# Gate logits with one load of the high half: 24 products a block in place of 36, and one more VectorE instruction

## The chip, the cores and the metric

The kernel runs on one core of one Trainium2 chip. The metric is the device time of one execution in microseconds. Five engines run side by side, each with a queue of its own: TensorE (PE in the rows, with its weight loads as PEld), VectorE (DVE), ScalarE (ACT), GpSimd (POOL) and SyncE (SP, which here only issues DMAs). They meet through semaphores alone.

## The reference, cut to what matters

Three layers follow each other: a linear attention over 4 x 8 heads, an MLP over 2304 rows (512 to 2048 to 512), and a mixture of 8 experts of which each row uses one. The change is in the gate of the third layer, which reads the MLP's result `x` (2304 x 512):

```
logits = x @ w_gate                                  # 512 x 8
e_idx  = argmax(logits, axis=1)
probs  = softmax(logits)                             # with + 1e-09 in the divisor
gate_w = probs[row, e_idx]
eom    = 1 / (1 + exp(-(x @ w_output_gate)))         # 512 x 8
out[row] = gate_w * eom[row, e_idx] * (relu(x[row] @ w1[e]) @ w2[e])     # e = e_idx[row]
```

Both small matrices lie side by side in the kernel, so that a row has 2 x 8 = 16 gate columns.

## The kernel before, in words

**Numbers as two halves.** float32 operands of the large products are split into two float16 halves, a high one and what is left of it, the low one. A product of two such operands is three products: high by high, high by low, low by high (`PARTS = ((0, 0), (0, 1), (1, 0))`, L328). For the gate, `yt` holds the transposed rows in both halves, `wg_sb` the 16 gate columns in both.

**The MLP's blocks.** The 2304 rows go in `BLOCKS` = 6 blocks of 384 rows (`BT` = 3 row tiles of 128). In `mlp_block` each block has 16 steps f, one for each 128 columns of the hidden layer. On TensorE a step is `hidden` two steps ahead (12 products of 384 columns, L898) and `output` (9 products of 512 columns, L909). Between them ScalarE makes a relu (L1249), VectorE the gated product (`gate_chunk`, L1650), ScalarE its high half (L1260), and VectorE its low half (`gate_lo`, L1655), for which `output` waits. TensorE needs VectorE's result two `hidden` calls later.

**What VectorE has beside it.** In the same steps VectorE prepares the experts' weights, three units of 128 x 4096 words a block: `unit_search` (L1569), `unit_scale` (L1584 to L1587) and `unit_lo` (L1594). ScalarE makes the units' high halves (L1237) and its queue waits for `unit_scale` before the first of them. At the end of a block VectorE finds the rows' largest values (`row_scales`, L1534 to L1542), and early in the next it makes the rows' low halves (L1561).

**The gate.** A block's gate is worked out within the next block: `y_logits(n - 1)` on TensorE after the `output` of step 8 (L925 to L940), `route_first` on VectorE in step 10 (L1607 to L1623), `ranks` on TensorE after the `output` of step 10 (L942), `route_second` on VectorE in step 12 (L1625 to L1645). In the last block of the MLP these come two steps sooner. The gate of the last block itself stands between the first two expert tiles. The order within each engine's queue is written out by hand. Blocks 1 to 4 are a loop of two blocks a turn, with 0 and 5 outside it.

Every instruction of the two route functions adds one to the semaphore `route` and the next waits for it; `ROUTE` is the count of a block, `ONEHOT` and `ARGS` are the counts at which `ranks` and ScalarE's two exponentials may start (L72, L943, L1226). All gate results lie in PSUM bank 7 (`LB`): 48 columns of logits from column 0, the ranks from column 128.

**After the MLP** come up to 27 tiles of 128 rows, each through its expert: `slot_hidden` (L994, 96 products of 128 columns) and `slot_output` (L1006, 24 products of 512 columns).

The functions in which the change lies:

Of the kernel before, what the change touches and what calls it, by code (L numbers as in the profile page):

```python
# [22 lines left out]
ALU = mybir.AluOpType  # L23
RMAX = bass.bass_isa.ReduceOp.max
ACT = mybir.ActivationFunctionType
AX = mybir.AxisListType

P = 128
# [3 lines left out]
E, EF = 8, 1024  # L32
# [10 lines left out]
BT = 3  # L43
BLOCKS = TILES // BT
BN = BT * P
DC = DM // P
# [22 lines left out]
SOON = (0, 1, 2, FC - 1)  # L69
W_UP = 3  # L70
YSTEPS, YUP = 6, 4
ONEHOT, ARGS, ROUTE = 6, 8, 21  # L72
NOWHERE = 2 * N


def moe_program(nc, qkt_in, v, w_phi, w_in, w_out, w_gate, w_ogate, w1, w2, out, rows, split, recs):
    ctx = ExitStack()

    def sb(name, shape, dt=F32):
        return ctx.enter_context(nc.sbuf_tensor(name, shape, dt))  # L80
# [4 lines left out]
    with ctx:  # L85

        ps = ctx.enter_context(nc.psum_tensor("ps", [P, 8, 512], F32))
# [3 lines left out]
        wg_sb = sb("wg_sb", [P, 2, DC, 2 * E], F16)  # L91
# [75 lines left out]
        yt = y_words[:, 0:DC * BN].bitcast(F16).rearrange("p (l c n) -> p l c n", l=2, c=DC)  # L167
# [26 lines left out]
        y_log = sb("y_log", [P, BT])  # L194
# [3 lines left out]
        lg = sb("lg", [P, BT, 2 * E])  # L198
# [129 lines left out]
        PARTS = ((0, 0), (0, 1), (1, 0))  # L328
# [8 lines left out]
        YB, HB, XB, LB = 0, (3, 4, 5), 6, 7  # L337
# [385 lines left out]
        def _(pe):  # L723
# [201 lines left out]
            def y_logits(n):  # L925

                if isinstance(n, int) and n == BLOCKS - 1:
                    pe.wait_ge(yt_ready, DC)
                else:
                    pe.wait_ge(yt_turned, n * (16 * BT) + 16 * BT)  # L930
                if not isinstance(n, int) or n == 0:
                    pe.wait_ge(low_copied, PAIRS)
                    pe.wait_ge(high_copied, PAIRS)
                pe.wait_ge(route, n * ROUTE + 1)
                for r in range(BT):
                    for c in range(DC):
                        for ly, lw in PARTS:
                            last = nc.tensor.matmul(ps[:, LB, r * 2 * E:(r + 1) * 2 * E], yt[:, ly, c, r * P:(r + 1) * P], wg_sb[:, lw, c, :],
                                                    start=c == 0 and ly + lw == 0, stop=c == DC - 1 and ly == 1)
                last.then_inc(logits_done, 1)  # L940

            def ranks(n):  # L942
# [5 lines left out]
            def mlp_block(n, a, post, more=True, ahead=0):  # L948
                first = isinstance(n, int) and n == 0
                pe.wait_ge(xs_hi, n + 1)  # L950
                pe.wait_ge(xs_lo, n + 1)
                if first:
                    pe.wait_ge(consts_made, 2)
                    pe.wait_ge(piece_hi, PAIRS // 2 - 1)
                    pe.wait_ge(piece_lo, PAIRS // 2 - 1)
                    pe.wait_ge(piece_hi_out, PAIRS // 2 - 2)
                    pe.wait_ge(piece_lo_out, PAIRS // 2 - 2)
                hidden(n, a, 0)
                hidden(n, a, 1)
                for f in range(FC):  # L960
                    if first and f + 2 == FC // 2:
                        pe.wait_ge(piece_hi, PAIRS // 2)
                        pe.wait_ge(piece_lo, PAIRS // 2)
                        pe.wait_ge(piece_hi_out, PAIRS // 2)
                        pe.wait_ge(piece_lo_out, PAIRS // 2)
                    if f + 2 < FC:
                        hidden(n, a, f + 2)
                    if not more and f == FC - 1:
                        pe.wait_ge(pos_ready, BLOCKS - 1)
                        for s in range(2):  # L970
                            slot_transposes(s, s, 1, (XB, LB)[s])
                    output(n, f)
                    if post and f == Y_AT + 5 - ahead:
                        y_logits(n - 1)
                    if post and f == Y_AT + 7 - ahead:
                        ranks(n - 1)
# [40 lines left out]
            n = BLOCKS - 1  # L1017
# [11 lines left out]
            pe.wait_ge(yt_ready, 1)  # L1029
            slot_output(0, 0, 0, (0,))  # L1030
            y_logits(n)
            slot_output(0, 0, 0, (1,))
            ranks(n)
# [269 lines left out]
        def _(dve):  # L1303
# [293 lines left out]
            def linker(start):  # L1597

                at = [start]

                def link(n, ins):
                    at[0] += 1
                    ins.then_inc(route, 1)
                    dve.wait_ge(route, n * ROUTE + (1 + at[0]))
                return link, at

            def route_first(n):  # L1607

                link, at = linker(0)
                dve.wait_ge(logits_done, n + 1)  # L1610
                link(n, nc.vector.tensor_tensor(lg[:], ps[:, LB, 0:BT * 2 * E].rearrange("p (r e) -> p r e", r=BT),
                                                y_log[:, :, None].to_broadcast([P, BT, 2 * E]), ALU.mult))
                link(n, nc.vector.tensor_reduce(r_mx[:], lg[:, :, 0:E], AX.X, ALU.max))
                link(n, nc.vector.tensor_tensor(r_a[:], lg[:, :, 0:E], r_mx[:, :, None].to_broadcast([P, BT, E]), ALU.subtract))

                link(n, nc.vector.scalar_tensor_tensor(out=r_b[:], in0=r_a[:], scalar=0.0, in1=iota8[:], op0=ALU.is_ge, op1=ALU.mult))
                link(n, nc.vector.tensor_reduce(r_s[:, 1, :], r_b[:], AX.X, ALU.min))
                link(n, nc.vector.tensor_tensor(onehot[:], iota8[:], r_s[:, 1, :, None].to_broadcast([P, BT, E]), ALU.is_equal))
                assert at[0] == ONEHOT
                link(n, nc.vector.tensor_tensor(r_b[:], onehot[:], lg[:, :, E:2 * E], ALU.mult))  # L1620
                link(n, nc.vector.tensor_reduce(r_s[:, 0, :], r_b[:], AX.X, ALU.add))
                assert at[0] == ARGS
                link(n, nc.vector.tensor_copy(yrow_words[:, :, DM + 1].bitcast(I32), token[:, bass.ds(n * BT, BT)]))  # L1623
# [70 lines left out]
            def mlp_block(n, a, post, units=3, ahead=0):  # L1694
                for f in range(FC):
# [37 lines left out]
                    if post and f == Y_AT + 7 - ahead:  # L1733
                        route_first(n - 1)
# [45 lines left out]
            slot_lo(0, 0, (3, 2))  # L1780
            slot_in(2, 0)
            route_first(BLOCKS - 1)
            route_second(BLOCKS - 1)
            slot_out(0, 0, None)
# [5 lines left out]
            def link(ins):  # L1790
                made[0] += 1
                ins.then_inc(table_step, 1)
                dve.wait_ge(table_step, made[0])
# [103 lines left out]
```

## Time and profile before

| | |
|---|---|
| median of 3 runs | 830.22 us (828.48 to 830.37) |
| the profiled execution | 827.24 us |
| its span, first to last instruction | 825.6 us |
| granted TensorE clock, mean | 0.996 |
| TensorE busy | 802.2 us (97%) |
| VectorE busy | 560.5 us (68%) |
| ScalarE busy | 393.0 us (48%) |

The span is cut into the attention (up to about 185 us), the MLP's blocks (185 to 567 us) and the experts' tiles. A busy share is a mean over all three. In 40 slices of about 20.6 us each, VectorE is at eight or nine tenths through the MLP's part, and below four tenths in most slices after it.

### The profile page before, as it was taken

What the parts mean: (1) busy time and instruction counts of PE and PEld (TensorE: products, weight loads), DVE (VectorE), ACT (ScalarE), POOL (GpSimd) and SP (SyncE); (2) the same over time, 40 slices, a digit from 0 to 9 for tenths busy, and PEclk for the clock granted to TensorE, in tenths of its full rate; (3) what the DMA queues carried; (4) which work ended last, traced back from release to release, by engine and by line L of the source; (5) the groups of instructions that cost most, each with busy time, mean ns of one, the idle gap of its engine ahead of it and who ended that gap; (6) DMA issues with size and microseconds to landing.
All of it is one profiled execution on the core that took longest, in us unless ns stands there. A gap on an engine that the chain in (4) does not pass through costs nothing.

```text
span 825.6 us, 19432 instructions
## 1 busy us (share of the span) xinstructions
PE 802.2 (97%) x7126; PEld 496.9 (60%) x7127; DVE 560.5 (68%) x1140; ACT 393.0 (48%) x857; POOL 179.9 (22%) x204
## 2 busy tenths in 40 slices
PE   7999999999999999999999999999999999999995
PEld 5666656655555555555555555556767777777773
DVE  5788798897978988888898897845723453222221
ACT  5888898883644644645646546434101121001110
POOL 4556666660000001010000001010211322111100
PEclk9999999999999999999999999999999999999998
DMA  7466677746656656855764756383273926266600
GB/s 237 148 204 206 213 237 207 215 143 219 233 204 217 228 206 220 262 210 207 217 253 167 246 219 208 135 343 142 83 278 142 378 65 237 78 231 248 235 28 14
DMA packets 67449, 164.37 MB, mean 199 GB/s; under 512 B 28614, under 2 KB 32966, under 8 KB 60736
## 3 DMA queue, kind: packets, MB, share of 16 engines
q1 hardware_dynamic: 61472, 146.74, 52.4%
q0 software_dynamic: 5760, 16.80, 5.7%
q8 instruction: 36, 0.59, 0.3%
q14 instruction: 21, 0.17, 0.1%
q10 hardware_dynamic: 160, 0.07, 0.0%
HBM read 114.16 MB, written 47.55 MB: 196 GB/s over the span
## 4 chain that ended last, share of the span: by engine, by line
PE 67%; DVE 16%; issue 10%; ACT 4%; DMA 1%; POOL 1%; SPq 1%; DVEq 0%; ACTq 0%; POOLq 0%
PE ps L909 17%; PE ps L898 15%; PE ps L994 11%; PE ps L1006 11%; PE ps L747 3%; DVE u_mx L1569 3%; DVE arena L1594 2%; PE ps L777 2%; PE ps L810 2%; DVE y_words L1561 1%; DVE arena L1320 1%; DVE arena L1337 1%; DVE relu L1650 1%; PE ps L984 1%; ACT arena L1112 1%
## 5 line engine op out<-in xcount | busy, mean ns | idle before, releaser
L898 PE MATMUL ps<-arena,w_in_sb 128*128 128x384 f16 x1152 | 200.9, 326 | 0.0
L909 PE MATMUL ps<-w_out_sb,arena 128*128 128x512 f16 x576 | 171.3, 379 | 1.5 <-DVE stage L1655 1.5
L898 PEld LDWEIGHTS ps<-arena,w_in_sb 128*128 128x128 f16 x1152 | 111.8, 98 | 81.1 <-issue 0.2
L1288 ACT ACTIVATE x_t<-ps 128x512 f16<-128x512 f32 x54 | 31.6, 596 | 200.3 <-PE ps L994 175.0
L994 PE MATMUL ps<-x_t,arena 128*128 128x128 f16 x2112 | 121.5, 219 | 2.0 <-issue 1.9
L994 PEld LDWEIGHTS ps<-x_t,arena 128*128 128x128 f16 x2112 | 119.2, 98 | 5.9 <-issue 2.6
L1006 PE MATMUL ps<-arena,x_t 128*128 128x512 f16 x528 | 117.9, 379 | 0.0
L909 PE MATMUL ps<-w_out_sb,stage 128*128 128x512 f16 x288 | 109.1, 379 | 0.0
L1260 ACT ACTIVATE arena<-relu 128x384 f16<-128x384 f32 x96 | 50.0, 521 | 119.1 <-DVE relu L1650 119.1
L909 PEld LDWEIGHTS ps<-w_out_sb,arena 128*128 128x128 f16 x576 | 55.7, 98 | 61.9 <-issue 4.8
L1762 DVE SCALAR_TENSOR_TENSOR x_t<-ps,x_t 128x512 f16<-128x512 f32 x54 | 36.7, 690 | 78.9 <-ACT x_t L1288 78.9
L1112 ACT ACTIVATE arena<-ps,arena 128x128 f32<-128x128 f32 x288 | 80.3, 386 | 12.9 <-DVE arena L1317 12.9
L1249 ACT ACTIVATE relu<-ps,three,s_h 128x384 f32<-128x384 f32 x96 | 63.4, 661 | 46.0 <-PE ps L898 45.8
L1006 PEld LDWEIGHTS ps<-arena,x_t 128*128 128x128 f16 x528 | 50.6, 98 | 56.7
L591 POOL TENSOR_TENSOR arena<-arena 128x512 f32<-128x512 f32 (+1 forms) x64 | 69.1, 1080 | 61.9 <-ACT arena L1112 57.4
L1594 DVE SCALAR_TENSOR_TENSOR arena<-arena,u_up 128x1024 f16<-128x1024 f32 x64 | 79.3, 1281 | 4.6 <-ACT arena L1237 4.6
L1237 ACT ACTIVATE arena<-arena,u_up 128x1024 f16<-128x1024 f32 x64 | 72.5, 1140 | 5.7 <-DVE u_up L1586 5.6
L1569 DVE TENSOR_REDUCE u_mx<-arena 128x1 f32<-128x1024 f32 x64 | 74.9, 1212 | 0.0
L641 POOL PARTITION_ALL_REDUCE u_all<-u_red x16 | 7.8, 489 | 298.3 <-DVE u_red L1573 298.3
L1650 DVE SCALAR_TENSOR_TENSOR relu<-relu,ps 128x384 f32<-128x384 f32 x96 | 52.8, 550 | 25.8 <-ACT relu L1249 25.5
L1772 DVE TENSOR_SCALAR x_t<-ps,stage 128x512 f32<-128x512 f32 x27 | 20.2, 749 | 68.7 <-PE ps L1006 68.7
L1655 DVE SCALAR_TENSOR_TENSOR stage<-relu,arena 128x384 f16<-128x384 f32 x96 | 53.1, 554 | 18.9 <-ACT arena L1260 18.6
(203 smaller groups left out, 892.0 us busy)
## 6 DMA issues: line engine op xcount, KB each, us to landing
arena<-split SPq DMA_DIRECT2D x36, 1024.0 KB
arena<-in_moe_w SPq DMA_DIRECT2D x16, 2048.0 KB
split<-arena SPq DMA_DIRECT2D x16, 2048.0 KB, 7.4
arena<-in_qkt SPq DMA_DIRECT2D x15, 576.0 KB, 6.3
stage<-in_moe_w_in SPq DMA_DIRECT2D x16, 512.0 KB, 5.3
stage<-in_moe_w_out SPq DMA_DIRECT2D x16, 512.0 KB, 6.1
x_t<-rows POOLq DMA_DIRECT2D x27, 257.0 KB
y_words<-recs SPq DMA_DIRECT2D x32, 144.0 KB, 3.0
```

The source lines that it names most:

```text
L591: nc.gpsimd.tensor_tensor(out, x, y, ALU.add).then_inc(sum_step, 1)
L898: last = nc.tensor.matmul(ps[:, HB[f % GB], 0:BN], w_in_sb[:, lw, c, f * P:(f + 1) * P], xt[:, a, lx, c, :], start=c == 0 and lw + lx == 0 ...
L909: last = nc.tensor.matmul(ps[:, YB + r, :], g_sb[lg_][:, f % GB, r * P:(r + 1) * P], w_out_sb[:, lw, f, :], start=f == 0 and lg_ + lw == 0 ...
L994: last = nc.tensor.matmul(ps[:, bank, f % 4 * P:(f % 4 + 1) * P], w1_sb[b][:, lw, c, f * P:(f + 1) * P], xgt[:, a, lx, c, :], start=c == 0 ...
L1006: last = nc.tensor.matmul(ps[:, 6 + a, :], hg[:, a, lh, f, :], w2_sb[b][:, lw, f, :], start=f == 0 and lh + lw == 0, stop=f == EFC - 1 and ...
L1112: last = nc.scalar.activation(pk[:, t0 + t, s, :], ps[:, bank, t * F:(t + 1) * F], ACT.Exp, bias=bias[:, t0 + t:t0 + t + 1], scale=1.0 - 2 ...
L1237: nc.scalar.activation(split_sb[:, 0, q_ * Q:(q_ + 1) * Q], raw[b][:, q_ * Q:(q_ + 1) * Q], ACT.Copy, scale=u_up[:, b:b + 1]).then_inc(u_h ...
L1249: nc.scalar.activation(relu3[:, f % GB, :], ps[:, HB[f % GB], 0:BN], ACT.Relu, bias=three[:, 0:1], scale=s_h[:, 0:1]).then_inc(relu3_ready, 1)
L1569: nc.vector.tensor_reduce(u_mx[:, q_:q_ + 1], raw[b][:, q_ * Q:(q_ + 1) * Q], AX.X, ALU.max, apply_absolute_value=True).then_inc(u_searche ...
L1594: nc.vector.scalar_tensor_tensor(out=split_sb[:, 1, cols], in0=raw[b][:, cols], scalar=u_up[:, b:b + 1], in1=split_sb[:, 0, cols], op0=ALU ...
L1650: nc.vector.scalar_tensor_tensor(out=relu3[:, f % GB, :], in0=relu3[:, f % GB, :], scalar=6.0, in1=ps[:, HB[f % GB], 0:BN], op0=ALU.min, o ...
L1655: nc.vector.scalar_tensor_tensor(out=g_sb[1][:, f % GB, :], in0=relu3[:, f % GB, :], scalar=CG / 6.0, in1=g_sb[0][:, f % GB, :], op0=ALU.m ...
```

## The change: what it does

`y_logits` gives TensorE the two halves of the gate's columns in one moving operand. For each row tile r and each 128 rows c of the model dimension the high half of `yt` is loaded once and multiplied by 32 columns, high and low gate weights side by side, and the low half of `yt` is loaded once and multiplied by the 16 high ones. These go into the first 16 of the tile's 32 PSUM columns. So there are 3 x 4 x 2 = 24 products a block where there were 36. The 16 columns of the high-by-low product are no longer added to the others by TensorE: a new first instruction of `route_first` adds the two groups of 16 columns, for 3 row tiles, from PSUM into `lg`. The multiplication by `y_log`, which read PSUM before, now reads and writes `lg`. The three counts of the semaphore `route` grow by one.

```diff
-ONEHOT, ARGS, ROUTE = 6, 8, 21
+ONEHOT, ARGS, ROUTE = 7, 9, 22
...
                 for r in range(BT):
+                    o = r * 4 * E
                     for c in range(DC):
-                        for ly, lw in PARTS:
-                            last = nc.tensor.matmul(ps[:, LB, r * 2 * E:(r + 1) * 2 * E], yt[:, ly, c, r * P:(r + 1) * P], wg_sb[:, lw, c, :],
-                                                    start=c == 0 and ly + lw == 0, stop=c == DC - 1 and ly == 1)
+                        rows_ = yt[:, :, c, r * P:(r + 1) * P]
+                        if c > 0:
+                            nc.tensor.matmul(ps[:, LB, o:o + 2 * E], rows_[:, 1], wg_sb[:, 0, c, :], start=False, stop=False)
+                        last = nc.tensor.matmul(ps[:, LB, o:o + 4 * E].rearrange("p (l e) -> p l e", l=2), rows_[:, 0], wg_sb[:, :, c, :],
+                                                start=c == 0, stop=c == DC - 1)
+                        if c == 0:
+                            nc.tensor.matmul(ps[:, LB, o:o + 2 * E], rows_[:, 1], wg_sb[:, 0, c, :], start=False, stop=False)
                 last.then_inc(logits_done, 1)
...
-                link(n, nc.vector.tensor_tensor(lg[:], ps[:, LB, 0:BT * 2 * E].rearrange("p (r e) -> p r e", r=BT),
-                                                y_log[:, :, None].to_broadcast([P, BT, 2 * E]), ALU.mult))
+                link(n, nc.vector.tensor_reduce(lg[:], ps[:, LB, 0:BT * 4 * E].rearrange("p (r l e) -> p r e l", r=BT, l=2), AX.X, ALU.add))
+                link(n, nc.vector.tensor_tensor(lg[:], lg[:], y_log[:, :, None].to_broadcast([P, BT, 2 * E]), ALU.mult))
```

## Rows read from the trace of the kernel before

**Rows 1.** The page's first part: busy us (share of the span), instructions.

```profile
PE 802.2 (97%) x7126; PEld 496.9 (60%) x7127; DVE 560.5 (68%) x1140; ACT 393.0 (48%) x857; POOL 179.9 (22%) x204
```

**Rows 2.** Busy time by stretch: us, then PE, PEld, DVE, ACT, POOL, clock, DMA share, GB/s.

```profile
265.28:329.22 63.94, 63.53 (x374) 33.70 (x375) 56.19 (x106) 35.64 (x53) 5.73 (x7) 1.00 0.64 216
329.22:392.88 63.66, 63.40 (x374) 33.69 (x375) 56.04 (x106) 35.52 (x53) 4.44 (x7) 1.00 0.69 230
...
520.24:567.00 46.76, 46.76 (x294) 25.20 (x295) 26.20 (x81) 17.69 (x29) 4.73 (x7) 1.00 0.53 209
```

**Rows 3.** TensorE's waits, 180 to 565 us: total us, times, longest.

```profile
PE ps L909 <- DVE stage L1655: 1.5, 5, 0.4
```

**Rows 4.** The chain of waits through block 1: start us, us, what.

```profile
286.68 1.15 DVE arena L1594
...
289.16 0.13 DVE lg L1611
...
329.22 2.10 PE ps L909 x9
331.32 1.95 PE ps L898 x12
```

**Rows 5.** The chain of waits, from block 2 into block 3.

```profile
348.84 1.94 PE ps L909 x9
350.79 0.89 PE ps L938 x36
...
377.08 0.68 ACT relu L1249
```

**Rows 6.** The gate's products, all of them: duration min/median/max ns, first and last start.

```profile
L938 PE MATMUL ps<-wg_sb,y_words x216: 169/169/173, 286.7 to 578.1; 128*128 128x16 f16 x108
```

**Rows 7.** VectorE's groups, shapes apart: busy us, mean ns | idle before.

```profile
L1320 DVE TENSOR_REDUCE arena<-ps 128x4 f32<-128x512 f32 x32 | 22.0, 687 | 18.8 <-PE ps L747 18.8
L1337 DVE TENSOR_REDUCE arena<-ps 128x2 f32<-128x256 f32 x16 | 6.7, 421 | 10.0 <-PE ps L747 9.9
L1819 DVE TENSOR_REDUCE stage<-stage 128x24 f32<-128x192 f32 x1 | 0.4, 353 | 0.0
```

**Rows 8.** VectorE in order of time, in blocks 1 and 2.

```profile
289.08 0.20 DVE L1611 TENSOR_TENSOR lg<-ps,y_log 128x48 f32<-128x48 f32 x1
289.31 0.18 DVE L1613 TENSOR_REDUCE r_mx<-lg 128x3 f32<-128x24 f32 x1
...
313.79 0.18 DVE L1542 RECIPROCAL y_up<-y_inv 128x3 f32<-128x3 f32 x1
314.10 0.55 DVE L1650 SCALAR_TENSOR_TENSOR relu<-relu,ps 128x384 f32<-128x384 f32 x1
...
370.80 0.56 DVE L1650 SCALAR_TENSOR_TENSOR relu<-relu,ps 128x384 f32<-128x384 f32 x1 [1.11 <-ACT relu L1249]
...
377.46 0.17 DVE L1542 RECIPROCAL y_up<-y_inv 128x3 f32<-128x3 f32 x1
377.80 0.55 DVE L1650 SCALAR_TENSOR_TENSOR relu<-relu,ps 128x384 f32<-128x384 f32 x1 [0.16 <-ACT relu L1249]
```

**Rows 9.** ScalarE in order of time, step 14 of block 2.

```profile
369.06 1.15 ACT L1237 ACTIVATE arena<-arena,u_up 128x1024 f16<-128x1024 f32 x1
```

**Rows 10.** VectorE in order of time, at the ends of blocks 3 and 4.

```profile
441.13 0.17 DVE L1542 RECIPROCAL y_up<-y_inv 128x3 f32<-128x3 f32 x1
441.44 0.55 DVE L1650 SCALAR_TENSOR_TENSOR relu<-relu,ps 128x384 f32<-128x384 f32 x1
...
504.76 0.17 DVE L1542 RECIPROCAL y_up<-y_inv 128x3 f32<-128x3 f32 x1
505.15 0.56 DVE L1650 SCALAR_TENSOR_TENSOR relu<-relu,ps 128x384 f32<-128x384 f32 x1 [0.22 <-ACT relu L1249]
```

**Rows 11.** The chain of waits in block 5 and at the experts' first tiles.

```profile
534.02 0.89 PE ps L938 x36
...
577.41 0.89 PE ps L938 x36
```

## The prediction, made before the changed kernel ran

> **What bounds the kernel now.** I read the page first [rows 1]: TensorE is busy for 97% of the span, VectorE for 68%. That says "TensorE", but it is a mean over three stages. So I cut the MLP's part at the points where TensorE was last held up, once a block [rows 2]. Blocks 1 and 2 take 63.9 and 63.7 us (3 and 4 are alike), and in such a stretch VectorE has 56 us of work: 88%, not 68%. In the last stretch it has 26.2 of 46.8 us, and TensorE never pauses. The list of TensorE's waits [rows 3] names one partner in the MLP, VectorE's `gate_lo`: five waits, 1.5 us in all. The cuts of rows 2 are where they end, at `output` of step 3.
>
> The chain of waits says what leads to those five points, and here blocks differ. In block 1 [rows 4] it leaves TensorE before the gate's products, enters VectorE at 286.68, passes through `route_first` (L1611 at 289.16) and stays on VectorE and on ScalarE waiting for VectorE until TensorE is released at 329.22. In block 2 [rows 5] it stays on TensorE, through the 36 products, and leaves it only at the next block's first relu (377.08). The reader is to see that these are two paths of almost one length, both closed by the same wait. The change shortens one and lengthens the other.
>
> **TensorE's side.** The 36 products took 0.89 us on the chain, 24.7 ns each [rows 5], though each lasts 169 ns from end to end [rows 6]: they overlap. 12 fewer is 12 x 24.7 = 0.30 us. Another 12 grow from 16 to 32 columns. No row has a 32-column product in a stream. From the large ones: 12 products of 384 columns go at 1.95 us (162.5 ns each) [rows 4], 9 of 512 at 1.94 us (215.6 ns) [rows 5]; that is 0.415 ns a column, so 32 columns would come to 162.5 - 352 x 0.415 = 16 ns, below the 24.7 ns that 16 columns take. So something other than columns paces these small products, and I take growth at nothing; the other bound is 12 x 16 x 0.415 = 0.08 us. TensorE gains 0.30 us a block (0.22 to 0.30, and nothing if loads pace it in another way), 1.8 us over six blocks.
>
> The trace shows 24.7 ns for a load with its product [rows 5]. The Trainium skill, "TensorE: Matmul & The Clock Gate", "Back-to-back issue gap", gives about 60 cycles for any product of 1 to 64 columns, and by that rule the gain is the same 0.30 us. The same page under "LDWEIGHTS" gives columns / 1.2 ns for a load, 107 ns for 128: if loads were paid in full, 12 fewer would give 1.3 us a block. The trace disagrees, 36 loads and products fitted in 0.89 us.
>
> **VectorE's side.** One instruction is added, and the chain of semaphores between them makes it cost a whole step. It reads 96 words of PSUM in groups of two. The rows have reductions from PSUM of 512 words at 687 ns and of 256 at 421 ns [rows 7]: 1.04 ns a word, so 96 words come to 421 - 160 x 1.04 = 255 ns. From one link's start to the next is 20 to 30 ns more than the duration (L1611 lasts 0.20, the next starts 0.23 later [rows 8]). I take 0.28 us. The bounds: 0.22 us, the step of the 24-word reduction after it, and 0.38 us, that of 192 words (353 ns [rows 7]). The multiplication keeps its 48 words and its 0.20 us; that it reads SBUF now I price at nothing. Behind the added instruction in VectorE's queue stand the rest of `route_first`, then `gate_lo` of step 10; ranks and exponentials shift by as much and nobody waits for them.
>
> The Trainium skill, "VectorE: DVE Perf Modes", "The perf-mode tier table", lets a reduction run at one element a cycle only. The 1.04 ns a word of rows 7 agrees.
>
> **Does 0.28 us reach the end of VectorE's path?** In steps 13 to 15 VectorE idles 1.11 us before a relu [rows 8], which looks like cover. It is not: ScalarE's queue is behind the weights' scale there. It starts L1237 at 369.06 [rows 9], as soon as VectorE has made the scale, makes the relu after it, and VectorE waits for that. A later VectorE makes ScalarE later, and the idle time only moves. The slack that counts is at the next block's first `gate_chunk`, where the relu comes from TensorE's side. In block 2 VectorE has 0.16 us idle before it [rows 8]. But in block 1, where nothing outside is late, the same step (end of L1542 at 313.97 to 314.10) takes 0.13 us anyway, so of the 377.63 to 377.80 of block 2 only 0.17 - 0.13 = 0.04 us is true slack. The same subtraction at the ends of blocks 3 and 4 [rows 10] gives 441.44 - 441.30 - 0.13 = 0.01 and 505.15 - 504.93 - 0.13 = 0.09 us. The other end is the whole gap as slack, 0.17, 0.14 and 0.22 us; I take the small ones, since block 1 is this very step.
>
> Block by block, the longer path decides:
> - Block 1 is on VectorE's path already: +0.28.
> - Blocks 2, 3, 4: VectorE's path is +0.28 less slack: +0.24, +0.27, +0.19. TensorE's is -0.30, and what it gains there is spent waiting for `gate_lo`.
> - Block 5, which works out block 4's gate: no unit of weights is left after the first, VectorE has 26.2 of 46.8 us of work [rows 2], TensorE's 0.89 us stands on the chain [rows 11]: -0.30.
> - The last gate, at 577.41, is on the chain as well [rows 11]. Behind it, ahead of `ranks`, stand 12 expert products of 512 columns, 12 x 215.6 ns = 2.6 us, which cover the longer `route_first`: -0.30.
>
> The sum is 0.98 - 0.60 = +0.38 us. The experts' tiles that follow start from TensorE's progress and shift with it. The profiled execution took 827.24 us, 1.6 us more than its span of 825.6, and by the sum would take 827.6. It lies 3.0 us below the median of the runs shown, 830.22, so the same sum on the median is 830.6 us. What a measurement of this kernel can tell from no change is about 0.3%, 2.5 us: the forecast is **no change**, with the sum slightly on the slow side.
>
> **Rivals.**
> 1. *TensorE is the bound throughout, as its 97% suggests.* Then VectorE's 0.28 us vanishes in its idle time (the 1.11 us of rows 8 speak for it, block 1's chain against), and 6 x 0.30 = 1.8 us are gained: 828.4 us. With slacks of 0.17, 0.14 and 0.22 and the cheap 0.22 us, it would still be +0.22 + 0.05 + 0.08 + 0 - 0.60 = -0.25, 830.0 us. 10%.
> 2. *VectorE's added step costs a multiple, so the kernel gets slower.* The place is the new reduction: 48 results of two words, 16 columns apart, from PSUM. Every reduction in the rows has groups of 8 or more words per result. Were each result to cost something of its own, say the whole to take twice 0.28, blocks 1 to 4 would give 0.56 + 0.52 + 0.55 + 0.47 = 2.1, less 0.60: +1.5, 831.7 us. It decides, that is passes 2.5 us, from a step of about (2.5 + 0.6 + 0.14) / 4 = 0.8 us. For it: two words a group is outside the rows. Against it: a reduction of 24 words in 3 groups takes 0.18 us [rows 8] and one of 192 in 24 groups 353 ns [rows 7], which is 1.04 ns a word again and no sign of a price per group. 14%.
> 3. *The products don't become cheaper.* If the pace is set by accumulating into the same PSUM columns, or a load is still issued for each of 36, TensorE gains nothing: 0.98, 831.2 us. The 24.7 ns were already reached with three products into the same columns, and the edit has one load and one product for each half. 8%.
> 4. *Something that I don't trace shifts by microseconds* (DMA order among the experts' tiles, code loading): either sign, 8%.
>
> **How the numbers follow.** The forecast holds 60%; it and rivals 1 to 3 all lie between 828.4 and 831.7 us, less than 0.3% from the median. The range takes in these ends and the runs' own spread of 828.48 to 830.37: 827.8 to 832.6 us. Within 0.3%: the 60%, nearly all of rivals 1 and 3, most of 2, half of 4: 87%. Slower: the costly end of rival 2 and part of 4, 8%. Faster: part of 4 and a little of 1, 5%.
>
> **What would show it.** In the changed profile: the gate's group has 144 products in place of 216, and the chain or timeline shows 24 of them in 0.59 us; a new reduction of about 0.25 us ahead of the multiplication, with 0.28 us between their starts. TensorE's waits for `gate_lo` in blocks 1 to 4 grow from 0.3 us each by 0.5 to 0.6 (some of it may show at step 12 or 15 already), and the chain runs on VectorE through the route functions in all four blocks, not in block 1 alone. The stretches of rows 2 become some 64.2, 63.9, 63.9 and 63.9 us, and the last 46.5. Should the waits stay as they are and the stretches shorten to 63.3, VectorE had slack and rival 1 is right. It is all wrong if the time moves by over 2.5 us, or if a wait appears anywhere outside these places.

## The result, and the profile after

| | before | changed |
|---|---|---|
| median | 829.49 us (15 runs, 828.07 to 832.37) | 831.61 us (15 runs, 830.65 to 834.31) |
| ratio | | 1.0022, 95% interval 1.0011 to 1.0032 |
| profiled execution, span | 825.6 us | 829.5 us |

The change costs 1.8 us (0.9 to 2.7): by the bound set ahead of the run no change, but clear of zero, and on the slow side. The forecast was +0.4. The two profiled spans differ by 3.9 us, but 3.1 of that stand ahead of the MLP's first cut (265.28 us before, 268.40 now), in a part that the change doesn't touch; it has its own line at the end. So the reading goes by blocks.

First the blocks, cut at the same events as [rows 2]. The columns are those of rows 2: the stretch, its length, then busy time of PE, PEld, DVE, ACT and POOL, clock, DMA share, GB/s.

```profile
268.40:332.49 64.09, 63.41 (x362) 33.32 (x363) 56.28 (x107) 35.52 (x53) 4.79 (x7) 1.00 0.64 216
332.49:397.89 65.40, 63.59 (x362) 33.16 (x363) 56.35 (x107) 35.54 (x53) 4.45 (x7) 1.00 0.66 224
397.89:461.97 64.08, 63.42 (x362) 33.31 (x363) 56.27 (x107) 35.52 (x53) 4.45 (x7) 1.00 0.61 214
461.97:525.96 63.99, 63.42 (x362) 33.29 (x363) 56.26 (x107) 35.55 (x53) 4.45 (x7) 1.00 0.67 215
525.96:572.44 46.48, 46.48 (x283) 24.89 (x284) 26.37 (x82) 17.70 (x29) 4.75 (x7) 1.00 0.54 210
```

TensorE has 12 products fewer in each block (x362 for x374), VectorE one instruction more (x107 for x106). The last stretch got shorter, 46.48 us against 46.76 before. The four above it got longer: by 0.15, 1.74, 0.44 and 0.27 us. Block 2 doesn't fit the others.

TensorE's waits in the MLP, where [rows 3] had five, 1.5 us (total, times, longest):

```profile
PE ps L909 <- DVE stage L1660: 3.9, 12, 1.3
```

The chain of waits in block 2 (start us, us, what), where [rows 5] had TensorE's 36 products and nothing of VectorE:

```profile
350.16 1.96 PE ps L898 x12
...
356.38 0.18 DVE lg L1616
...
356.58 0.22 DVE lg L1617
...
378.77 1.25 issue
380.02 0.08 DVEq L1748
```

The reader is to see two things. The chain now runs through the sum (L1616) and the multiplication in block 2 too, as it did in block 1 before [rows 4]. And there is something that no part of the sum had: 1.25 us in which VectorE waits for nothing that the profile shows, in its queue at L1748, which is the loop of blocks 1 to 4 (L1743 before). VectorE in order of time there, and the DMA queues from 372 to 386 us (queue, kind: packets, MB, share of 16 engines):

```profile
376.30 2.48 DVE L1599 SCALAR_TENSOR_TENSOR arena<-arena,u_up 128x1024 f16<-128x1024 f32 x2
380.16 0.69 DVE L1539 TENSOR_REDUCE y_mx<-ps 128x1 f32<-128x512 f32 x1 [1.39 <-issue]
```

```profile
q1 hardware_dynamic: 590, 1.18, 21.7%
q0 software_dynamic: 240, 0.79, 14.0%
q14 instruction: 3, 0.02, 0.7%
q8 instruction: 1, 0.02, 0.6%
```

The first instruction after the jump back to the loop's start comes 1.39 us late. Before the change the same two instructions follow each other without a pause, and no packet of q14 or q8, the queues of kind "instruction", falls into these 14 us. Over the whole span q14 (the "second instruction queue" of the expectations) has 26 packets for 21. The one packet of q8 doesn't belong to the pause: e1, e3, e8 and e9 below have the pause without it, e6 and e11 have it without the pause.

### The profile page after: what moved, and what is told of

It is laid out like the page before. It is cut to its first block, busy times and chain, and to the rows that moved or that the text cites. A ratio compares the mean times of both kernels' runs of the same rounds, so it can differ in the third digit from the quotient of the medians.

```text
span 829.5 us, 19298 instructions
## 1 busy us (share of the span) xinstructions
PE 802.1 (97%) x7054; PEld 494.1 (60%) x7055; DVE 561.9 (68%) x1146; ACT 393.2 (47%) x857; POOL 180.7 (22%) x204
## 4 chain that ended last, share of the span: by engine, by line
PE 59%; DVE 21%; issue 12%; ACT 5%; POOL 1%; DMA 0%; DVEq 0%; ACTq 0%; POOLq 0%
PE ps L909 12%; PE ps L898 12%; PE ps L999 11%; PE ps L1011 11%; DVE u_mx L1574 4%; PE ps L747 4%; DVE arena L1599 3%; PE ps L777 2%; PE ps L810 2%; DVE relu L1655 2%; DVE arena L1342 2%; DVE y_words L1566 1%; DVE arena L1325 1%; PE ps L989 1%; DVE stage L1660 1%
```

## The experiments

Each kernel below was timed in 5 rounds against the kernel before, e4 to e7 on another chip than the rest. Block times are cut as in rows 2, from one profiled execution each; q14 is the packets of that queue over the span.

| run | block 1 | 2 | 3 | 4 | q14 | ratio (95%) |
|---|---|---|---|---|---|---|
| before, first trace | 63.94 | 63.66 | 63.64 | 63.72 | 21 | |
| e0 before | 63.83 | 63.66 | 63.64 | 63.72 | 21 | 1.0008 (0.9993 to 1.0022) |
| changed, first trace | 64.09 | 65.40 | 64.08 | 63.99 | 26 | 1.0022 (1.0011 to 1.0032) |
| e1 changed | 64.29 | 65.70 | 64.08 | 63.97 | 26 | 1.0042 (1.0025 to 1.0059) |
| e2 TensorE's part | 64.17 | 63.63 | 63.61 | 63.68 | 21 | 1.0000 (0.9986 to 1.0015) |
| e3 VectorE's part | 64.14 | 65.39 | 64.06 | 63.98 | 26 | 1.0032 (1.0016 to 1.0049) |
| e4 one idle copy | 63.81 | 63.66 | 63.64 | 63.71 | 21 | 0.9990 (0.9976 to 1.0004) |
| e5 changed, no 1e-09 | 63.98 | 63.72 | 63.69 | 63.76 | 21 | 0.9988 (0.9973 to 1.0002) |
| e6 changed, lean | 63.88 | 63.45 | 63.44 | 63.51 | 20 | 0.9973 (0.9958 to 0.9988) |
| e7 before, lean | 63.77 | 63.76 | 63.74 | 63.81 | 20 | 1.0019 (1.0000 to 1.0038) |
| e8 two idle copies | 63.82 | 65.13 | 63.75 | 63.71 | 26 | 1.0016 (1.0000 to 1.0033) |
| e9 copies ahead of the loop | 63.68 | 65.09 | 63.63 | 63.72 | 26 | 1.0009 (0.9993 to 1.0025) |
| e10 sum three times | 64.65 | 65.13 | 64.53 | 64.54 | 26 | 1.0025 (1.0010 to 1.0040) |
| e11 changed, lean, again | 63.89 | 63.45 | 63.44 | 63.50 | 20 | 0.9964 (0.9946 to 0.9981) |

The whole times of one kernel lie 3.7 to 7.3 us apart between its fastest and its slowest execution; in the three kernels that were traced twice, blocks 3 and 4 repeat within 0.02 us, and there the experiments speak.

**e0 and e1: both kernels again.**

> The kernel before, unchanged, as the measure of what two runs of one program differ by. Expected ratio 1.000 within 0.001. For the traces: theory A (the changed kernel's 1.3 us hold-up of VectorE without a releaser, at the loop turn behind block 2, belongs to the longer program) expects none of over 0.5 us here; theory B (it comes and goes from run to run, whatever the program) gives it an even chance of standing here too. The same for TensorE's pause ahead of the last attention pair's column sums (0.8 us in the trace of before, 2.4 in that of after).

> The changed kernel again. Ratio 1.001 to 1.003. Theory A expects the same hold-up of about 1.3 us at the loop turn, so block 2 takes 65.4 us again; theory B expects 64.1 us, like blocks 1, 3 and 4, or the hold-up in another place.

Theory A held. The hold-up of 1.4 us (1.7 in e1) stood at the same place in both traces of the changed kernel and in neither of the kernel before. TensorE's pause near 180 us was 0.80 us in the first trace of before and 2.41 in e0: that one comes and goes with the run and is not the change's.

**e2: TensorE's part alone.**

```diff
-link(n, nc.vector.tensor_reduce(lg[:], ps[:, LB, 0:BT * 4 * E].rearrange("p (r l e) -> p r e l", r=BT, l=2), AX.X, ALU.add))
-link(n, nc.vector.tensor_tensor(lg[:], lg[:], y_log[:, :, None].to_broadcast([P, BT, 2 * E]), ALU.mult))
+link(n, nc.vector.tensor_tensor(lg[:], ps[:, LB, 0:BT * 4 * E].rearrange("p (r l e) -> p r l e", r=BT, l=2)[:, :, 0, :],
+                                y_log[:, :, None].to_broadcast([P, BT, 2 * E]), ALU.mult))
```

> 24 products, but no sum: the high-by-low products are computed and left out of the logits, so VectorE has the instructions of the kernel before. Two-path theory: blocks 1 to 4 stay at 63.6 to 63.9 us (VectorE closes them), the last MLP block and the last gate give 0.30 us each: 0.6 to 0.8 us gained in all. Rival (TensorE is the bound throughout): 0.30 us in each of six blocks, 1.8 us gained, blocks 2 to 4 at 63.35 us.

Blocks 2 to 4 shrank by 0.03 to 0.04 us where TensorE had 0.30 less to do: the rival, for which they had to come to 63.35, is out. Block 1 grew by 0.23 us, which neither side expected; it is the block that varies (see the account of the prediction). The whole time shows no gain within its interval of 1.2 us to either side, too wide for the 0.6 expected; in the trace, the way from the last cut to block 5's transposes (L921) took 52.70 us against 52.99 before, as forecast for block 5.

**e3: VectorE's part alone.** 36 products, the four high-by-low ones of a row tile in a group of their own.

```diff
+for ly in range(2):
+    nc.tensor.matmul(ps[:, LB, o:o + 2 * E], yt[:, ly, c, r * P:(r + 1) * P], wg_sb[:, 0, c, :],
+                     start=c == 0 and ly == 0, stop=c == DC - 1 and ly == 1)
...
+last = nc.tensor.matmul(ps[:, LB, o + 2 * E:o + 4 * E], yt[:, 0, c, r * P:(r + 1) * P], wg_sb[:, 1, c, :],
+                        start=c == 0, stop=c == DC - 1)
```

> 36 products of 16 columns as before, but the high-by-low ones into columns of their own, and VectorE's sum as in the change. Two-path theory: blocks 1 to 4 at 63.9 to 64.1 us, as in the changed kernel, because TensorE's 0.30 us did not count there; the last block and the last gate as before: 0.9 to 1.0 us slower in all. Rival (VectorE's step is hidden and the changed kernel's loss is something else): no change within 0.3 us in any block.

Blocks 3 and 4 at 64.06 and 63.98 us are those of the changed kernel (64.08, 63.99): in these blocks the 24 products are worth nothing (the kernel that has them is even 0.01 to 0.02 us the longer). The hold-up came too, with 36 products, so it belongs to VectorE's program.

**e4, e8 and e9: what the hold-up hangs on.** All three are the kernel before with copies of one word (`pad`) that nothing waits for. e4 and e8 have one and two a block in VectorE's idle time before the last step, so that its program's loop is 2 and 4 instructions longer (waits and register instructions counted; the change makes it 4 longer). e9 has four copies in block 0, ahead of the loop.

```diff
+if post and f == FC - 1:                # e8; e4 has one copy
+    for j_ in range(2):
+        nc.vector.tensor_copy(pad[:, j_:j_ + 1], three[:])
...
+if not post and f == FC - 1:            # e9
+    for j_ in range(4):
+        nc.vector.tensor_copy(pad[:, j_:j_ + 1], three[:])
```

> The kernel before with one copy of a single word a block, on VectorE, unlinked, ahead of the last step's gated product, where VectorE idles 1.1 us; nothing waits for it. It makes the loop of blocks 1 to 4 longer by as many instructions as the change's sum does. Theory L (the changed kernel's 1.3 us at the loop turn come from the longer loop in VectorE's program, whose code has to be loaded again): VectorE held up 1.4 us without a releaser ahead of the rows' maximum behind the loop turn, block 2 at 65.0 to 65.4 us, 5 more packets on the second instruction queue (26 in place of 21), 1.2 us slower in all. Rival P (the hold-up belongs to the sum, or to VectorE being late): blocks 1 to 4 at 63.6 to 63.9 us, 21 packets, no change.

> The kernel before with two unlinked one-word copies a block in VectorE's idle time before the last step's product, so that its program between the loop's ends has as many instructions as in the changed kernel (the one copy a block of the run before gave half of that, and no hold-up). Theory L (code at the loop turn, with a threshold between the two lengths): a hold-up of about 1.4 us ahead of the rows' maximum behind the loop turn, 26 packets on the second instruction queue, block 2 at 65.0 us or more, the other blocks at 63.6 to 63.9 us, 1.2 us slower in all. Rival P (it belongs to the sum, or to VectorE being late): nothing moves, 21 packets.

> The kernel before with four one-word copies ahead of the loop, in block 0, and the loop itself unchanged. The loop's last instruction then has the place that it has in the changed kernel, its length is that of the kernel before. If what counts is the place where the loop ends: hold-up of 1.4 us, 26 packets, block 2 at 65.0 us. If what counts is the loop's length: none, 21 packets.

e4 spoke for rival P: nothing moved. I had taken one copy for as long as the sum, but the sum brings a register instruction with it, so e4 is half of the step. With the full step the hold-up came (e8), and it came just as well with the loop's length untouched and its end moved by as much (e9). This is read from one trace of each; by the whole times e8 is 1.3 us slower than the kernel before (0.0 to 2.7) and e9 0.7 (-0.6 to 2.1), which alone would not show it. Behind the loop turn of e9:

```profile
379.36 0.69 DVE L1535 TENSOR_REDUCE y_mx<-ps 128x1 f32<-128x512 f32 x1 [1.39 <-issue]
```

and of e4:

```profile
376.78 0.69 DVE L1535 TENSOR_REDUCE y_mx<-ps 128x1 f32<-128x512 f32 x1
```

So neither the sum nor the loop's length is the cause, but where in VectorE's program the loop ends: 2 instructions later than before is free, 4 later costs 1.4 us and 5 packets of code. Theory L was right on code and wrong on length. The Trainium skill, "Runtime: NRT & Kernel Launch", "Instruction fetch mechanics", says that an engine holds two pages of 256 instructions and that a taken branch whose target has left them waits for a DMA. The traces agree in kind: the pause stands right behind the jump back, with 3 packets of q14 from 372 to 386 us in e1, e3, e8, e9 and e10 as well and in none of the others.

The compiled programs fit, too. Counted from 0, the jump back is VectorE's instruction 762 in the kernel before, in e2 and in e5, 764 in e4, 751 in e6 and 747 in e7, all without the hold-up; it is 766 in the changed kernel, e3, e8 and e9, and 774 in e10, all with it. So if a page border decides, it lies at 765 or 766. The traces have a second mark some 256 instructions ahead of it: in block 1 the link that ends at VectorE's instruction 511 takes 0.36 to 0.38 us from start to start, where its neighbours take 0.21 to 0.22. In e6, e7 and e11, which have one instruction more ahead of the loop, it is the link that ends at 510, with 0.46 us. Only e9 and e10 don't have it. From the kernel before:

```profile
289.75 0.18 DVE L1616 SCALAR_TENSOR_TENSOR r_b<-r_a,iota 128x24 f32<-128x24 f32 x1
290.11 0.18 DVE L1617 TENSOR_REDUCE r_s<-r_b 128x3 f32<-128x24 f32 x1 [0.18 <-DVE r_b L1616]
```

In block 3, in the loop's second turn, the same link is late only in the changed kernel, e1, e3 and e8, all of them kernels with the hold-up at the jump. That both marks are page borders, at 510 and 766, is worked out from this and not tested by itself. The jump is taken once, behind block 2, so a kernel pays once.

**e5: the changed kernel without `+ 1e-9`**, which adds to a sum of at least 1.

```diff
-link(n, nc.vector.tensor_scalar(r_s[:, 2, :], r_s[:, 2, :], 1e-9, None, ALU.add))
```

> The changed kernel without the instruction that adds 1e-09 to a sum that is at least 1 (in float32 it changes nothing), so VectorE's loop has as many instructions as before the change, and its path is 0.20 us shorter than in the changed kernel. Theory L: no hold-up at the loop turn, 21 packets; blocks 1 to 4 at 63.85, 63.8, 63.8, 63.75 us, 2.1 us less than the changed kernel in all, and 0.2 us less than the kernel before. Rival P: the hold-up stays and block 2 takes 65.2 us.

As theory L expected: the sum is there, the loop ends where it did, no hold-up, 21 packets. Blocks 1 to 4 came to 63.98, 63.72, 63.69 and 63.76 us: 0.13 over the forecast, 0.08 and 0.11 under it, and 0.01 over. It is level with the kernel before within its interval.

**e6, e7 and e11: VectorE made shorter than TensorE.** Besides the 1e-09, four instructions of `route_second` become one, and `ranks` does the counting.

```diff
-nc.tensor.matmul(ps[:, LB, 128:128 + BT * E], tri16[:], rhs, start=True, stop=True)
-nc.tensor.matmul(ps[:, LB, 192:192 + BT * E], ones16[:], rhs, start=True, stop=True).then_inc(ranks_done, 1)
+for k in range(BT):          # hot: onehot behind two row tiles of zeros
+    nc.tensor.matmul(ps[:, LB, 128:128 + BT * E], (tri16, ones16, ones16)[k][:], rhs[:, (2 - k) * E:(2 - k + BT) * E],
+                     start=k == 0, stop=k == BT - 1)
+for r in range(BT):
+    last = nc.tensor.matmul(ps[:, LB, 192:192 + E], ones16[:], rhs[:, (2 + r) * E:(3 + r) * E], start=r == 0, stop=r == BT - 1)
...
-for r in range(BT):
-    link(n, nc.vector.tensor_tensor(base[:, r + 1, :], base[:, r, :], total[:, r, :], ALU.add))
-link(n, nc.vector.tensor_tensor(r_b[:], base[:, 0:BT, :], rank, ALU.add))
+link(n, nc.vector.tensor_tensor(r_b[:], base[:, 0:1, :].to_broadcast([P, BT, E]), rank, ALU.add))
...
-link(n, nc.vector.tensor_copy(base[:, 0, :], base[:, BT, :]))
+link(n, nc.vector.tensor_tensor(base[:, 0, :], base[:, 0, :], ps[:, LB, 192:192 + E], ALU.add))
```

> The change, without the 1e-09, and with the running counts of the row tiles summed by TensorE: 6 small products in place of 2 in the ranks, 4 instructions of VectorE less than in the changed kernel (0.8 us of its path). Two-path theory: VectorE's path is 0.5 us shorter than before the change, so TensorE closes blocks 2 to 4: each 63.66 - 0.30 + 0.10 = 63.46 us, block 1 the same; with 0.20 us each in the last two gates: 0.4 + 0.6 + 0.4 = 1.4 us gained against the kernel before. Theory L adds that no hold-up stands at the loop turn, as the loop is shorter. Rival (the 24 products give nothing in blocks 1 to 4 for another reason): blocks stay at 63.65 us.

> The same two savings of VectorE in the kernel before, with its 36 products. Two-path theory: TensorE closes blocks 1 to 4 already, so 0.8 us less on VectorE buys nothing and 4 more products of 25 ns cost 0.10 us a block: blocks at 63.75 us, no change or 0.3 us slower in all. If VectorE were the bound of those blocks, they would come to 62.9 us and 3 us would be gained.

> The lean version of the change once more, for its interval: ratio 0.996 to 0.999 to the kernel before, blocks 2 and 3 at 63.45 us, block 1 between 63.5 and 63.9 us.

The cleanest answer of all. Forecast for blocks 2 to 4 with the 24 products 63.46 us, measured 63.45, 63.44, 63.51; with 36 products 63.75, measured 63.76, 63.74, 63.81. Once VectorE's path is the shorter, the 12 products are worth 0.30 us a block, and the same cut in VectorE buys nothing without them. A stretch of e6 beside one of e7 (TensorE's 63.19 and 63.50 us busy are the difference):

```profile
328.87:392.32 63.45, 63.19 (x366) 33.52 (x367) 55.67 (x103) 35.64 (x53) 4.43 (x7) 1.00 0.69 229
```

```profile
328.94:392.70 63.76, 63.50 (x379) 33.88 (x379) 55.43 (x102) 35.74 (x53) 4.44 (x7) 1.00 0.66 230
```

e6 and e11 beat the kernel before, each on its own chip: 0.9973 and 0.9964, 2.2 us (1.0 to 3.5) and 3.0 us (1.6 to 4.5) less. The changed kernel was measured above 1 both times. Some 1.1 us of it can be followed: from the first cut to the last block's transposes (L921 before) both take 307.08 us, where the kernel before took 307.95 and in e0 307.85, and the last gate adds 0.2. The rest was not followed; nor was e7's whole time, 1.6 us over the kernel before (0.0 to 3.1), where its blocks give 0.1 to 0.2. Block 1 kept 63.88 us, with a wait of 0.69 us, which is why the 1.4 us expected didn't come in full. The traces show where it comes from: VectorE takes 0.41 us for L1552 (0.17 in block 2) and starts the second `gate_chunk` behind it (L1656 at 317.80) another 0.2 us late, and e11 has both at the same places. Why is open.

**e10: the slope.**

> The changed kernel with the sum made three times in a row, each linked to the next. Two-path theory: 0.56 us more in each of blocks 1 to 4 (64.6 us), block 2 with the hold-up besides (66.0), blocks 5 and the last gate as in the changed kernel: 2.2 us slower than the changed kernel. Rival (VectorE's step is partly hidden): less than 0.4 us a block.

Block 1 grew by 0.56, block 3 by 0.45, block 4 by 0.55 us: VectorE's steps count in full (block 3 lost the late link of 0.17 us that it has in the changed kernel). Block 2 took less than expected, since the hold-up was 0.56 us here in place of 1.39, with the same 26 packets. How much of a code load shows differs, then; here the jump stands 8 instructions further than in the changed kernel, and whether that is why is open. By blocks the kernel is 1.3 us slower than the changed one, where 2.2 were expected; the ratio, 1.0025, can't be told from the changed kernel's two, 1.0022 and 1.0042.

## Why the prediction was right, and what it missed

- *TensorE gains 0.30 us a block, growth at nothing.* Right. On the chain the last gate's 24 products run from 582.83 to 583.43 us, 0.60 us for 0.89 [rows 11]: 25 ns each, 16 or 32 columns alike. The last MLP stretch gave 0.28 us.
- *VectorE's sum is a step of 0.28 us.* Right: VectorE in order of time in block 3, with 0.29 us between the starts of the sum and the multiplication.

```profile
421.69 0.25 DVE L1616 TENSOR_REDUCE lg<-ps 128x48 f32<-128x96 f32 x1
421.98 0.21 DVE L1617 TENSOR_TENSOR lg<-lg,y_log 128x48 f32<-128x48 f32 x1
422.22 0.18 DVE L1618 TENSOR_REDUCE r_mx<-lg 128x3 f32<-128x24 f32 x1
422.43 0.18 DVE L1619 TENSOR_TENSOR r_a<-lg,r_mx 128x24 f32<-128x24 f32 x1
422.81 0.18 DVE L1621 SCALAR_TENSOR_TENSOR r_b<-r_a,iota 128x24 f32<-128x24 f32 x1 [0.19 <-DVE r_a L1619]
```

- *The 0.16 us of idle time are mostly no slack.* Right for size. Forecast for blocks 1 to 4: 0.28, 0.24, 0.27, 0.19; measured 0.15, (1.74), 0.44, 0.27. Block 1 varies (63.68 to 64.29 us over the runs other than e10): in the first trace of before L1540 took 0.30 us there, 0.17 in e0, and against e0's 63.83 it grew by 0.26. Block 3 holds an extra 0.17 us in one link (0.38 between the last two starts above, where links of its size have 0.21 to 0.22), repeated in e1 and e3, and in e8, which has no sum. It stands only where the hold-up does, so it goes with the code and not with the sum: 0.44 less 0.17 is the 0.27 forecast.
- *TensorE's gain is spent waiting in blocks 1 to 4.* Right, by e2 and e3, and by e6 against e7. Its waits on `gate_lo` went from 5 to 12, two or three a block where there was one: besides step 3, at steps 12 and 15, as the forecast had it. They grew from 1.5 to 3.9 us, some 1.0 of it at the hold-up; that leaves about 0.35 us a block by the list, less than the 0.5 to 0.6 forecast. The chain of block 2 now runs on VectorE through the route functions.
- *Rival 1 (TensorE bounds throughout)* fell with e2; *rival 2 (a price for each result of two words)* with 0.25 us for the sum; *rival 3* with the 24 products in 0.60 us.
- *The sum was +0.38.* Here the prediction missed a term. By blocks it is 0.15 + 1.74 + 0.44 + 0.27 - 0.28 - 0.29 = 2.0 us, which agrees with the 1.8 of the ratio, and some 1.45 of block 2's 1.74 are the code load at the loop turn (block 2 grew by 1.47 in e8 and 1.43 in e9, with no sum in them). Without it and the 0.17 of block 3 the blocks give 0.4, which is the sum as forecast. I had put code loading into rival 4 with half of 8%, as something that can't be traced. It could have been suspected: the program of an engine that closes every block was made longer inside a loop. Its size could not be read from the trace of before, which has no such pause at that place. The prediction had named a wait outside its places as a sign of being wrong: TensorE's waits all stand where it said, VectorE's 1.39 us at the jump do not.

The median stood 2.1 us over before and inside the range. The terms worked out were right in kind and near in size, but they are a fifth of what was measured; most of it was the term left out, and that it fell inside the range is luck: the range reached that far for rival 2 and for the spread of the runs, not for this.

## What to carry to other kernels

When two engines take turns at closing a loop, price an edit on each path to the same wait, and count idle time before a wait as slack only after taking off what the same step costs where nobody is late. A saving on one engine is worth nothing until the other's path is shorter; find out which instructions of the other can go, as the 1e-09 and the running counts here, and make both edits together. And an instruction added to a queue moves every later one: look at the first instruction behind each loop's jump, and at the packets of the code queues, before blaming the instruction itself.

## What the runs showed of the hardware that was not expected

- Four one-word copies that nobody waits for, ahead of a loop, cost 1.4 us at its turn (e9's trace; the whole time, 0.7 us with an interval from -0.6 to 2.1, is too wide to show it).
- In a stream of small products, 32 columns cost what 16 do: 25 ns with the weight load.
- TensorE's unexplained pause near 180 us was either 0.8 or 2.4 us, in runs of the same program. In seven of the eight traces with the long one the granted clock from 182 to 184 us was 0.50 to 0.72, where 0.50 is 1.2 GHz; in e4 it stayed 1.00. With the long pause the first cut of rows 2 stands at 267.06 to 271.02 us, with the short one at 264.99 to 266.87: a single execution moves by about 3 us, more than this change.
